# A rebuilt lead-in: one set of rotation tables, queries of the first pair turned by two engines, a bank for each transposed block, an order of its own for the first pair

## What is computed

```python
# q, k, v: [4, 8, 576, 64]
def rotate(x):
    x1, x2 = (x[..., :half], x[..., half:])
    return np.concatenate([x1 * cos - x2 * sin, x1 * sin + x2 * cos], axis=-1)
q_rot, k_rot = (rotate(q), rotate(k))
scores = np.matmul(q_rot, k_rot.transpose(0, 1, 3, 2)) / np.sqrt(D)
scores = scores - np.max(scores, axis=-1, keepdims=True)
attn = np.exp(scores)
attn = attn / (np.sum(attn, axis=-1, keepdims=True) + 1e-09)
x = np.matmul(attn, v)                      # then [2304, 512]
gate = 1.0 / (1.0 + np.exp(-(x @ w_gate)))  # [2304, 1536]
y = (gate * (x @ w_val)) @ w_out
h = y @ w_in                                # [2304, 1024]
out = layer_norm(h * softmax(h)) * g_ln @ w_out2
```

## Time and profile before

| | |
|---|---|
| median of 3 runs | 970.41 us (969.49 to 973.93) |
| the profiled execution | 973.27 us |
| its span | 971.5 us |
| TensorE busy | 941.3 us, 97% |
| VectorE, ScalarE, GpSimd busy | 52%, 37%, 35% |

### The profile page before, as it was taken

How to read it: one execution, slowest core, us unless ns; L and a number is a source line. 1 busy time by engine, 2 the same in 40 slices (tenths; PEclk the granted TensorE clock), 3 DMA queues, 4 the chain that set the end, 5 groups by cost and what they waited for, 6 DMA issues and landing times.

```text
span 971.5 us, 15365 instructions
## 1 busy us (share of the span) xinstructions
PE 941.3 (97%) x5392; PEld 788.7 (81%) x5392; DVE 507.8 (52%) x889; ACT 361.0 (37%) x778; POOL 343.0 (35%) x250
## 2 busy tenths in 40 slices
PE   2899999999999999999999999999999999999998
PEld 1788888888877789888888888888888888888886
DVE  4789889898973524233233233234434454444441
ACT  2778878787772211111110110110111243333332
POOL 5565756556402641500500500600774522222200
PEclk9999999999999999999999999999999999999999
DMA  4233323333230120100200100100111011000001
GB/s 124 62 90 96 85 76 91 82 91 85 73 103 1 65 66 1 66 1 1 65 1 1 65 1 0 43 0 0 43 46 41 0 22 23 22 22 22 22 22 44
DMA packets 32130, 42.78 MB, mean 44 GB/s; under 512 B 5728, under 2 KB 20448, under 8 KB 32096
## 3 DMA queue, kind: packets, MB, share of 16 engines
q1 hardware_dynamic: 32096, 42.32, 15.6%
HBM read 28.74 MB, written 4.72 MB: 34 GB/s over the span
## 4 chain that ended last, share of the span: by engine, by line
PE 93%; DVE 2%; issue 1%; DMA 1%; ACT 1%; POOL 1%; SPq 0%; POOLq 0%; DVEq 0%
PE ps L1065 30%; PE ps L1100 15%; PE ps L1163 10%; PE ps L1002 9%; PE ps L1047 8%; PE ps L1138 8%; PE ps L1029 8%; PE ps L973 2%; PE ps L1148 2%; DMA raw_w<-in_moe_w_out 1%; DMA g_sb<-in_moe_g_ln 0%; DVE qT L791 0%; POOL x_lo L654 0%; DVE nmax L817 0%; POOL w_lo L549 0%
## 5 line engine op out<-in xcount | busy, mean ns | idle before, releaser
L1065 PE MATMUL ps<-x_hi,w_hi 128*128 128x512 f32 (+1 forms) x480 | 177.1, 369 | 0.2 <-POOL w_lo L549 0.2
L1065 PE MATMUL ps<-x_lo,w_hi 128*128 128x512 f32 (+1 forms) x480 | 176.7, 368 | 0.0
L1065 PE MATMUL ps<-x_hi,w_lo 128*128 128x512 f32 (+1 forms) x480 | 176.6, 368 | 0.0
L884 DVE TENSOR_TENSOR hid<-ps,sig 128x512 f32<-128x512 f32 (+1 forms) x60 | 38.3, 638 | 234.7 <-PE ps L1065 206.8
L733 ACT ACTIVATE sig<-ps 128x512 f32<-128x512 f32 (+1 forms) x60 | 33.3, 555 | 295.0 <-PE ps L1065 295.0
L1002 PE MATMUL ps<-kT,qT 128*128 128x288 f32 (+2 forms) x672 | 124.9, 314 | 7.8 <-ACT prob L694 5.1
L817 DVE TENSOR_REDUCE nmax<-ps 128x1 f32<-128x576 f32 x144 | 108.7, 755 | 26.8 <-PE ps L1002 22.9
L593 POOL TENSOR_SCALAR w_hi<-raw_w 128x1024 fp32r<-128x1024 f32 x15 | 41.3, 2777 | 210.5 <-PE ps L1100 210.5
L694 ACT ACTIVATE prob<-ps,nmax 128x576 f32<-128x576 f32 x128 | 94.2, 739 | 51.5 <-DVE nmax L817 50.1
L1002 PEld LDWEIGHTS ps<-kT,qT 128*128 128x128 f32 x672 | 96.0, 194 | 16.9 <-issue 7.4
L1065 PEld LDWEIGHTS ps<-x_hi,w_hi 128*128 128x128 f32 x480 | 90.5, 189 | 16.1 <-issue 0.9
(11 more groups left out here) (109 smaller groups left out, 1638.6 us busy)
## 6 DMA issues: line engine op xcount, KB each, us to landing
kT<-kT SPq DMA_DIRECT2D x30, 288.0 KB, 4.0
raw_k<-in_k SPq DMA_DIRECT2D x16, 288.0 KB, 2.8
raw_q<-in_q SPq DMA_DIRECT2D x16, 288.0 KB, 3.1
out_y<-y_sb SPq DMA_DIRECT2D x36, 128.0 KB, 2.3
v_sb<-in_v SPq DMA_DIRECT2D x64, 64.0 KB, 2.3
raw_w<-in_moe_w_gate SPq DMA_DIRECT2D x6, 512.0 KB, 3.7
raw_w<-in_moe_w_val SPq DMA_DIRECT2D x6, 512.0 KB, 4.7
raw_w<-in_moe_w_out SPq DMA_DIRECT2D x6, 512.0 KB, 6.4
```

Of the source, the lines that this page charges most:

```text
L884: nc.vector.tensor_tensor(hid[:, f, 0:n], gv_ps[f][1][:, 0:n], sig[:, f, 0:n], ALU.mult).then_inc(hid_ready, 1)
L1065: last = nc.tensor.matmul(in_parts(gv_ps[f][n][:, 0:size(c)], c), w, x, start=m == 0, stop=m == len(todo) - 1)
```

## The change

Two tables are sent instead of four; ScalarE makes those of the queries with a scaled copy. ScalarE's queue sends cos and eye. The eye goes straight to its place (`eye_f`), without a cast. The first queries are rotated by VectorE (slots 0 to 3) and GpSimd (slots 4 to 8). The memsets stand ahead of the first rotation. Blocks k, T, q of pair 0 have banks 0, 1, 2 (LEAD) with semaphores of their own, and step -1 is gone. ScalarE's and VectorE's copies of these blocks are signalled one by one. Step 0 has its own lists (FIRST_PE, FIRST_ACT, FIRST_DVE). On SP, raw_q of pair 1 waits for VectorE's readings too (`q0_prod`), and g goes behind v. The diff, cut to its core:

```diff
-    of_keys = [np.ascontiguousarray(tiles(t), np.float32) for t in (cos, sin2)]
-    return [t * np.float32(D ** -0.5) for t in of_keys] + of_keys
+    return [np.ascontiguousarray(tiles(t), np.float32) for t in (cos, sin2)]
...
+        FIRST_PE = ["S0", "S1", "S2", "k", "S3", "T", "S4", "S5", "q", "B1", "S6", "B0", "S7", "A3", "S8"]
+        FIRST_ACT = ["S0", "S1", "S2", "k", "S3", "T", "S4", "S5", "q", "S6", "B0", "S7", "A3", "S8"]
+        FIRST_DVE = ["S0", "S1", "S2", "S3", "k", "S4", "T", "S5", "S6", "q", "B1", "S7", "S8"]
+        Q0_FIRST = 4
...
+        LEAD = {"k": 0, "T": 1, "q": 2}
...
 (SP)
             load(0, k, raw_k, k_in, k_prod)
-            for t, x in zip((cos_k, sin_k), rope[2:]):
-                sp.dma_start(t[:].rearrange("p t d -> p (t d)"), x).then_inc(rope_k_in, 16)
+            sp.dma_start(sin_k[:].rearrange("p t d -> p (t d)"), rope[1]).then_inc(sin_in, 16)
             load(0, q, raw_q, q_in, q_prod)
-            for t, x in zip((cos_q, sin_q), rope[:2]):
-                sp.dma_start(t[:].rearrange("p t d -> p (t d)"), x).then_inc(rope_q_in, 16)
-
-            sp.dma_start(prob[0][:, 0:P], eye).then_inc(const_in, 16)
-            sp.dma_start(g_sb[:], g_ln).then_inc(const_in, 16)
             load(1, k, raw_k, k_in, k_prod)
+            sp.wait_ge(q0_prod, 3)
             load(1, q, raw_q, q_in, q_prod)
             load_v(0)
+            sp.dma_start(g_sb[:], g_ln).then_inc(g_in, 16)
...
 (GpSimd)
+            def first_q():
+
+                s = slice(Q0_FIRST, SLOTS)
+                dst, src = (x[:, s, :].rearrange("p t (e d) -> p t e d", e=2) for x in (rot_q, raw_q))
+                cos = cos_q[:, s, :].unsqueeze(2).broadcast_to([P, SLOTS - Q0_FIRST, 2, HALF])
+                pool.wait_ge(q_in, 16)
+                pool.wait_ge(cos_q_ready, 1)
+                nc.gpsimd.tensor_tensor(dst, src, cos, ALU.mult).then_inc(q_prod, 1)
+                pool.wait_ge(sin_q_ready, 1)
+                for half in range(2):
+                    a, b = half * HALF, (1 - half) * HALF
+                    nc.gpsimd.tensor_tensor(swp[:, s, a:a + HALF], raw_q[:, s, b:b + HALF], sin_q[:, s, a:a + HALF],
+                                            ALU.mult).then_inc(q_prod, 1)
+                pool.wait_ge(q_prod, 3)
+                nc.gpsimd.tensor_tensor(rot_q[:, s, :], rot_q[:, s, :], swp[:, s, :], ALU.add).then_inc(q_rot, 1)
...
-            for name, p in (("RQ", 0), ("RK", 1)):
-                item(name, p, -1)
+            first_q()
+            pool.wait_ge(sin_in, 16)
+            pool.wait_ge(cos_in, 16)
+            item("RK", 1, -1)
...
 (ScalarE)
+            def first_tables():
+
+                for src, dst, arrived, ready in ((cos_k, cos_q, cos_in, cos_q_ready), (sin_k, sin_q, sin_in, sin_q_ready)):
+                    act.wait_ge(arrived, 16)
+                    nc.scalar.activation(dst[:], src[:], ACT.Copy, scale=D ** -0.5).then_inc(ready, 1)
+
+            def first_hi(name, full, done):
+
+                act.wait_ge(full, 1)
+                for dst, src, rows in hi_parts(name, tr_ps[LEAD[name]], 0, kT):
+                    nc.scalar.activation(dst[rows], src[rows], ACT.Copy).then_inc(done, 1)
+
+            def first_swapped(name, done):
+
+                for n, (dst, src, rows) in enumerate(of_keys(name, kTs)):
+                    if name == "k":
+                        act.wait_ge(k0_lo, n + 1)
+                    nc.scalar.activation(dst[other_half(rows)], src[rows], ACT.Copy).then_inc(done, 1)
+
+            act.dma_start(cos_k[:].rearrange("p t d -> p (t d)"), rope[0]).then_inc(cos_in, 16)
+            act.dma_start(eye_f, eye).then_inc(eye_in, 16)
+            first_tables()
+            first_hi("k", k0_turned, k0_hi)
+            first_swapped("k", k0_swapped)
+            first_hi("T", t0_turned, t0_hi)
+            first_swapped("T", t0_swapped)
+            first_hi("q", q0_turned, q0_hi)
+            pipeline(act, ORDER_ACT, item, FIRST_ACT)
...
 (VectorE)
-            first_k()
-            dve.wait_ge(const_in, 32)
-            nc.vector.tensor_copy(eye_r[:], prob[0][:, 0:P]).then_inc(eye_ready, 1)
...
+            first_rotation(raw_k, cos_k, sin_k, slice(0, SLOTS), x_f, k_in, (cos_in, 16), (sin_in, 16), rot_k, k_prod, k_rot)
+            first_rotation(raw_q, cos_q, sin_q, slice(0, Q0_FIRST), rrep, q_in, (cos_q_ready, 1), (sin_q_ready, 1),
+                           rot_q, q0_prod, q0_rot)
+            first_lo("k", k0_hi, k0_lo)
+            first_swapped("k", k0_swapped, k0_lo)
+            dve.wait_ge(t0_swapped, 1)
+            first_lo("T", t0_hi, t0_lo)
+            first_swapped("T", t0_swapped, t0_lo)
+            first_lo("q", q0_hi, q0_lo)
...
 (TensorE)
-            pe.wait_ge(eye_ready, 3)
-            pe.wait_ge(tails_clear, 5)
+            pe.wait_ge(eye_in, 16)
...
+            pe.wait_ge(k_rot, 1)
+            turn_pieces("k", LEAD["k"]).then_inc(k0_turned, 1)
+            pe.wait_ge(q_rot, 1)
+            turn_pieces("T", LEAD["T"]).then_inc(t0_turned, 1)
+            pe.wait_ge(q0_rot, 1)
+            turn_pieces("q", LEAD["q"]).then_inc(q0_turned, 1)
+            pipeline(pe, ORDER_PE, item, FIRST_PE)
```

More of the change, by code:

```diff
@@ L283, in use @@
             if isinstance(step, int):
-                return bank, sum(exists(owner(n, s)) for s in range(-1, step + 1) for n in mine
+                return bank, sum(exists(owner(n, s)) for s in range(0, step + 1) for n in mine
                                  if s < step or mine.index(n) < mine.index(name))
@@ L301, in steps_of, with pipeline @@
                     item(name, p, step)
-        def pipeline(eng, order, item):
-            for step in range(2):
-                steps_of(order, step, item)
+        def pipeline(eng, order, item, first=None):
+            steps_of(first or order, 0, item)
+            steps_of(order, 1, item)
             with eng.Fori(1, PAIRS // 2 - 1) as j:
@@ L569, in item @@
                 if name == "RQ":
[L570 removed]
+                    rotate(p, raw_q, cos_q, sin_q, q_in, rot_q, q_prod, q_rot, k_rot, num(p) + 1,
+                           ("q", "T", q0_turned, t0_turned))
                 elif name == "RK":
[L572 removed]
+                    rotate(p, raw_k, cos_k, sin_k, k_in, rot_k, k_prod, k_rot, q_rot, num(p),
+                           ("k", "T", k0_turned, t0_turned))
                 elif name == "XL":
@@ L772, in _, with first_rotation @@
         def _(dve):
[L773 to L778, removed]
+            def first_rotation(raw, cos, sin, slots, tmp, arrived, cos_done, sin_done, rot, prod, done):
+                dst, src = (x[:, slots, :].rearrange("p t (e d) -> p t e d", e=2) for x in (rot, raw))
+                tmp = tmp[:].rearrange("p (t d) -> p t d", t=SLOTS)[:, slots, :]
+                n = slots.stop - slots.start
+                dve.wait_ge(arrived, 16)
+                dve.wait_ge(*cos_done)
+                nc.vector.tensor_tensor(dst, src, cos[:, slots, :].unsqueeze(2).broadcast_to([P, n, 2, HALF]),
+                                        ALU.mult).then_inc(prod, 1)
+                dve.wait_ge(*sin_done)
@@ L779, in first_k @@
                 for half in range(2):
                     a, b = half * HALF, (1 - half) * HALF
[L781 to L784, removed]
+                    nc.vector.tensor_tensor(tmp[:, :, a:a + HALF], raw[:, slots, b:b + HALF], sin[:, slots, a:a + HALF],
+                                            ALU.mult).then_inc(prod, 1)
@@ L790, in qk_lo @@
                 for dst, src, rows in hi_parts(name, tr_ps[bank], par(p), kT):
                     last = nc.vector.tensor_tensor(dst[other_half(rows)], src[rows], dst[rows].bitcast(F32), ALU.subtract)
-                if step == -1 and name in "kT":
-                    pairs = zip(hi_parts(name, tr_ps[bank], par(p), kT), hi_parts(name, tr_ps[bank], par(p), kTs))
-                    for (hi, src, rows), (dst, _, _) in list(pairs)[-2 + (name == "T"):]:
-                        last = nc.vector.tensor_tensor(dst[rows], src[rows], hi[rows].bitcast(F32), ALU.subtract)
@@ L1186 @@
     inputs["moe2_g_ln"] = np.asarray(inputs["moe2_g_ln"]).reshape(KT2, P).T
-    given = [(n, inputs[n]) for n in _INS] + list(zip(("cos_q", "sin_q", "cos_k", "sin_k"), rope)) + [("eye", np.eye(P, dtype=np.float32))]
+    given = [(n, inputs[n]) for n in _INS] + list(zip(("cos", "sin"), rope)) + [("eye", np.eye(P, dtype=np.float32))]
     arrays, args = {}, []
```

68 lines of the change are left out of this document (42 added, 26 removed).

## The result

The changed kernel takes 963.51 us (median of 4 runs, 963.04 to 964.37) beside 970.81 us for the kernel before (969.49 to 973.93): ratio 0.9921, interval 0.9896 to 0.9946. That is 7.3 us; 6.2 were forecast, and 964.2 for the median. A second set, five runs of the changed kernel on another occasion, gave 964.09 beside 970.59, ratio 0.9933 (0.9919 to 0.9946), 6.5 us.

What follows compares the result with a forecast made beforehand. The prediction took TensorE's full stream as the bound, its late beginning as the gain: 6.15 (start) + 0.4 (order) - 0.35 (pace) = 6.2 us, from a median of 970.41 to 964.2, range 961.3 to 967.3.

Steps and rivals of the forecast that it cites:

- The mechanism and the sum: Lead-in before TensorE's full stream: gain is how much earlier that stream begins, 6.15 + 0.4 - 0.35 = 6.2 us.
- S8: Last score tile of pair 0, taken as the full stream's beginning: forecast at 30.95 us instead of 37.17.
- Transfers: Start of the lead-in: with two tables fewer, sin lands at 5.1 us, q near 6.45, keys rotated at 6.75.
- Taking turns: First queries' rotation: VectorE and GpSimd serialise on SBUF reads, 2.85 + 1.27 us, both through near 10.5.
- The chain on ScalarE and VectorE: Copies of transposed blocks k, T, q after VectorE's release at 10.5: first score at 15.5, 6.15 us earlier.
- Step 0: First score to last score tile of pair 0: new lists bring 0.4 us, TensorE's pace, doubling 11.2 us in, costs 0.35.
- Side by side: First queries' rotation: both engines run without conflict, first score at 13.4, 962.1 us; chance 0.12.
- Half pace into the full stream: TensorE's pace doubles only in the full stream, 2 to 6 us after S8: gain 3.7, 966.7 us; chance 0.17.
- S8 held by pair 1's rotations: S8 hangs on pair 1's rotations or transfers, not the first score: gain 1 to 4 us, 968; chance 0.05.

Runs made afterwards that it cites:

- pool_all: Changed kernel with GpSimd alone rotating all nine slots of the first queries, VectorE none: 963.94 us (single run).
- vector_all: Changed kernel with VectorE alone rotating all nine slots of the first queries, GpSimd none: 963.19 us (single run).
- all_three_old_lists: Changed kernel with VectorE alone rotating first queries, later gate-weight casts, TensorE fillers in lead-in and step 0, but old step 0 lists: median 959.44 us, ratio 0.9885.
- changed_again: The changed kernel without any edit, timed and profiled a second time: median 964.09 us beside 970.59 for the kernel before, ratio 0.9933.
- shared_bank: Changed kernel with blocks T and q of pair 0 sharing one bank again: 966.71 us (single run).
- four_tables: Changed kernel with four tables again, all sent from SP in the order of the kernel before: 966.36 us (single run).
- busy_pe: Changed kernel with 28 more transposes of the eye on TensorE in its waits of the lead-in: 964.65 us (single run).
- vector_all_late: vector_all with VectorE's first two casts of gate weights moved behind the maxima of S5 and S6 of the last pair: median 961.38 us, ratio 0.9898.

## Why the prediction was right, step by step

**The mechanism and the sum.** Right: the gain is that of an earlier full stream. The start was put at 6.15 us and was 6.67; S8 at 6.2 and was 7.7 and 6.8 in two profiles; 7.3 and 6.5 us by the medians. For the profiled execution 967.1 was forecast and 963.82 measured, 3.3 less; some 2 of it is the slow place near 290 us in the profile before, which the step to medians (2.9 us) took out. In the second profile the distance from the first score to S8 is 15.5, as forecast (30.95 - 15.5), but not for the reason given: one doubling some 11 us after the first score was assumed, and the pace doubled 6 us after it and fell back. That the number fits there is luck.

**Transfers.** Sin landed by 4.97 (forecast 5.1, between the 4.9 of an unchanged time from issue and the 5.6 by bytes). Eleven of the twelve profiles with these transfers have sin's first reader at 4.8 to 5.2 and pool_all at 5.67, so most are near the unchanged time and one is at the other value; no run changes the issuer alone. The mis-sized term was q: it was in by 5.8, not 6.45, some 4.1 us after its issue at 1.65. It landed just ahead of the keys' sum and not during it, and the sum was held up: keys at 7.28, not 6.75. On the path this cost nothing, because VectorE's part of the queries ended later still.

**Taking turns.** Right in kind: vector_all and pool_all show it from both sides (0.76 alone, 1.45 and 1.90 beside GpSimd). Wrong in size: the keys' sum and all eight operations took 3.87 us from 5.81 to 9.68, where the lengths that I had set add up to 4.8. Either the small operations are shorter than on my line or parts of them overlap; the runs do not separate the two. For the second speaks what the prediction read too roughly: an operation that had to wait did not end its own full length after the other's end. It ended 0.55 after it instead of 0.69 in the earlier trace rows (327.83 and 327.28), 0.61 instead of 0.76 in the changed kernel, 0.62 in pool_all. Some 0.14 less for each of seven or so turns would be the missing 0.9, an estimate. In pool_all the one that came second, by 0.12 us, waited for the whole of the first, which kept its 1.40. The Trainium skill ("SBUF — State Buffer", Who interferes with whom) says that the second engine blocks for the whole instruction of the first; the 1.90 of pool_all agrees. The sections of the change are worth 1.9 (bank) and 1.6 (tables) at the first score; the split is worth nothing against GpSimd alone as far as the one run tells, and costs 1.0 against VectorE alone (in four profiles of five; at S8 only 0.2 of it is left without fillers). If the two parts add, the other 3.2 of the 6.7 us (the eye without a cast, memsets ahead, copies signalled one by one, raw_q's place in the queue) were not undone one at a time.

**The chain on ScalarE and VectorE.** From VectorE's release to the first score 5.3 us (9.68 to 14.99), forecast 5.0. VectorE worked through in all of it, with gaps of 0.03 us between one group of copies and the next, as laid out; its copies took 1.41 where I had 1.38 to 1.39, T's a little more, and from its last copy's end to the score passed 0.14 (14.85 to 14.99), which I had at nothing.

**Step 0.** The layout by hand fits to 0.1 us with the pace put in afterwards: it gives 29.47 for a doubling at 22.5 and a start at 15.0, measured 29.45. For the old lists at full pace it was off by 1.1 (12.35, measured 13.5 in all_three_old_lists), where the pace fell. Its 0.4 us for the new lists was not shown: at the same early doubling the layout has the old ones 0.2 ahead. As the traces read, what the lists change is when TensorE works without a break, and so its pace; one run of the old lists at an untouched pace does not show it. Lists and pace together were to bring 0.05 us (0.4 less 0.35); they brought 1.0 in the first profile (distance 14.5 instead of 15.5) and nothing in the second (15.5). I had not forecast that the pace could fall back within step 0, which it did in six of the ten profiles of kernels without fillers in step 0: changed_again, vector_all, shared_bank, four_tables, busy_pe and vector_all_late.

**The rivals.** Side by side: refuted. Half pace into the full stream: not seen in any of the runs. S8 held by pair 1's rotations: no, TensorE never waited for GpSimd in step 0; the only waits on it are before T, in the lead-in.

## What to carry to other kernels

A short lead-in ahead of a full stream of TensorE work is worth its own microseconds and no more: find the first instruction of the full stream, and count an edit by how far it moves that one. Before splitting work between VectorE and GpSimd, look for operations of two SBUF inputs that grow beside each other; one engine alone may be through sooner. And where a wait-ridden stretch on TensorE precedes, idle slots filled with harmless transposes can be worth as much as a shorter chain, since the chain itself runs at TensorE's pace: here 1.6 us by the medians, beside 1.0 at the first score for the shorter chain. They are no guarantee; in all_three_old_lists the pace fell once with them.

## What the runs showed of the hardware that I had not expected

The pace of TensorE can be had before the first real score (1.29 us for eight score matmuls instead of 2.26, after 28 transposes of the eye that nobody reads), and it can be lost within the same step: the granted clock read 0.75 from 25 to 30 us in vector_all after waits of 0.75 and 1.10 us. The length of a wait does not decide alone: in the changed kernel's first profile TensorE waits 1.57 us before A3 (at 29.04) and keeps its pace. An earlier start that brought an earlier doubling (near 21 instead of near 22.7) ended nearly level, because the fall came with it.

The granted clock shows the fall but not the slow beginning. In changed_again it reads 1.00 from 15 to 20 us, where four score matmuls take 1.31 to 1.33 us, and 0.50 from 25 to 26 us, where they take the same 1.31:

```profile
15.00:20.00 5.00, 4.25 (x17) 3.88 (x18) 2.27 (x3) 1.66 (x4) 3.80 (x4) 1.00 0.35 105
25.00:26.00 1.00, 1.00 (x6) 1.00 (x6) 0.46 (x1) 0.51 (x2) 0.91 (x2) 0.50 0.28 65
```

So before the first doubling the pace is read from the length and spacing of equal matmuls, and only afterwards from the clock too.
